# Attention rounds beside Strassen passes: a round's transposes moved from the end of its own unit to the head of the next one, its mix one unit further

## The reference

```python
scores = scale * np.matmul(q_c, k_c.transpose(0, 1, 2, 4, 3))
scores = scores - np.max(scores, axis=-1, keepdims=True)
attn = np.exp(scores)
attn = attn / (np.sum(attn, axis=-1, keepdims=True) + 1e-09)
out = np.matmul(attn, v_c)
...
gate = 1.0 / (1.0 + np.exp(-(x @ w_gate)))      # 512 -> 1536
val = x @ w_val
x = (gate * val) @ w_out                        # 1536 -> 512
...
h = x @ w_in                                    # 512 -> 2048
g = np.where(h >= 1, h, np.where(h <= -1, 0.0, (h + 1) ** 2 / 4))
return g @ w_out                                # 2048 -> 512
```

## Time and profile before

| what | value |
|---|---|
| median of 3 runs | 1626.27 us (1622.51 to 1630.38) |
| the profiled execution, own time | 1621.38 us |
| its span | 1619.5 us |
| granted PE clock, mean | 1.00 |
| PE busy | 1595.8 us (99%) |
| DVE busy | 1138.2 us (70%) |
| ACT busy | 787.5 us (49%) |
| POOL busy | 513.3 us (32%) |

### The profile page before, as it was taken

The page is one execution under the profiler, slowest core; times in us unless marked ns, Lnnn a source line. Parts: engine busy times, 40 slices in busy tenths (PEclk is TensorE's granted clock), DMA queues, the critical chain, the costliest instruction groups (busy, mean ns, idle before and its releaser), DMA issues.

```text
span 1619.5 us, 29171 instructions
## 1 busy us (share of the span) xinstructions
PE 1595.8 (99%) x11174; PEld 1564.2 (97%) x11174; DVE 1138.2 (70%) x1611; ACT 787.5 (49%) x1269; POOL 513.3 (32%) x722
## 2 busy tenths in 40 slices
PE   8999999999999999999999999999999999999999
PEld 7899999999999999999999999999999999999998
DVE  5745667776695777678447579588688688588685
ACT  2222344534353444445334475575575575565663
POOL 7877844565765566566400000000000000000000
PEclk9999999999999999999999999999999999999999
DMA  9889799899999999989977877787778878777775
GB/s 304 290 290 331 265 379 358 311 350 368 328 334 363 344 333 322 353 332 325 349 284 262 284 291 284 248 307 278 261 295 285 275 290 275 282 296 257 258 279 170
DMA packets 135449, 489.50 MB, mean 302 GB/s; under 512 B 14224, under 2 KB 55696, under 8 KB 106256
## 3 DMA queue, kind: packets, MB, share of 16 engines
q1 hardware_dynamic: 106096, 417.24, 73.0%
q0 software_dynamic: 12032, 37.76, 6.0%
q10 hardware_dynamic: 17184, 32.64, 5.7%
HBM read 406.32 MB, written 81.26 MB: 301 GB/s over the span
## 4 chain that ended last, share of the span: by engine, by line
PE 85%; DVE 8%; DMA 3%; issue 2%; ACT 1%; POOL 1%; SPq 0%; DVEq 0%; ACTq 0%
PE banks L890 16%; PE banks L892 15%; PE banks L891 15%; PE banks L912 10%; PE banks L914 10%; PE banks L913 10%; DVE split_lo L1646 3%; PE banks L774 1%; PE banks L776 1%; PE banks L775 1%; PE banks L744 1%; DMA tile_in<-v_dram 1%; PE banks L765 1%; PE banks L753 1%; DMA stage_ab<-w_gate_dram 1%
## 5 line engine op out<-in xcount | busy, mean ns | idle before, releaser
L890 PE MATMUL banks<-combo_hi,ring 128*128 128x384 f32 x1512 | 512.4, 339 | 1.3 <-ACT chain L1174 1.1
L892 PE MATMUL banks<-combo_hi,ring 128*128 128x384 f32 x1512 | 505.5, 334 | 0.0
L891 PE MATMUL banks<-combo_lo,ring 128*128 128x384 f32 x1512 | 505.2, 334 | 0.0
L912 PE MATMUL banks<-split_hi,ring 128*128 128x384 f32 x1092 | 366.8, 336 | 5.9 <-DVE split_lo L1646 5.4
L914 PE MATMUL banks<-split_hi,ring 128*128 128x384 f32 x1092 | 365.1, 334 | 0.0
L913 PE MATMUL banks<-split_lo,ring 128*128 128x384 f32 x1092 | 365.0, 334 | 0.0
L890 PEld LDWEIGHTS banks<-combo_hi,ring 128*128 128x128 f32 x1512 | 283.8, 188 | 4.7 <-ACT chain L1174 1.4
L891 PEld LDWEIGHTS banks<-combo_lo,ring 128*128 128x128 f32 x1512 | 284.0, 188 | 0.0
L892 PEld LDWEIGHTS banks<-combo_hi,ring 128*128 128x128 f32 x1512 | 283.8, 188 | 0.0
L1174 ACT ACTIVATE chain<-banks 128x384 f32<-128x384 f32 x324 | 157.3, 488 | 246.0 <-PE banks L892 244.8
L1646 DVE TENSOR_TENSOR split_lo<-g,split_hi 128x768 fp32r<-128x768 f32 x234 | 237.7, 1020 | 32.3 <-ACT split_hi L1251 30.9
(11 more groups left out here) (131 smaller groups left out, 2130.6 us busy)
## 6 DMA issues: line engine op xcount, KB each, us to landing
ring<-w_out_split SPq DMA_DIRECT2D x119, 1024.0 KB, 5.8
ring<-w_in_split SPq DMA_DIRECT2D x108, 1024.0 KB, 6.3
ring<-w_in_split SPq DMA_DIRECT2D x108, 768.0 KB, 7.9
ring<-w_out_split SPq DMA_DIRECT2D x35, 512.0 KB, 5.7
tile_in<-q_k_dram ACTq DMA_DIRECT2D x43, 384.0 KB, 6.8
w_in_split<-weights SPq DMA_DIRECT2D x36, 256.0 KB, 4.0
x_raw<-x_scratch SPq DMA_DIRECT2D x6, 1536.0 KB, 8.9
out_dram<-y SPq DMA_DIRECT2D x24, 384.0 KB, 6.6
```

The costliest lines, as they stand in the source:

```text
L890: pe.matmul(ps, w_lo, hi, start=first and k == 0, stop=False, skip_group_check=more)
L891: pe.matmul(ps, w_hi, lo, start=False, stop=False, skip_group_check=more)
L892: last = pe.matmul(ps, w_hi, hi, start=False, stop=k == 1, skip_group_check=more)
L912: pe.matmul(ps[:, j, :], w_lo, hi, start=first and k == 0, stop=False, skip_group_check=more)
```

## The change

In a unit u of the passes 0 to 3, PE's list has now at its head: the scores of round u-1, the mix of round u-3 and the transposes of round u-2. Before, it had there the scores of round u-1 and the mix of round u-2, and the transposes of round u-1 between product 3 of the unit before and product 7. On ACT, save_x takes round u-3 in place of u-2 (units 3 to 10), and copy_probs_t round u-2 in place of u-1 (units 2 to 9), both at their old places in the unit. On DVE nothing moves. Two rounds are now under way with probabilities at once, so odd rounds use half of `out_chain2`, which is idle in the units. shift waits for the mix and the save of one round less, and the scores wait for the shift of the round before.

```diff
         def probs_of(a):
-            return early[:, a, 3 * N:4 * N] if a < EARLY else probs[:, :]
+            if a < EARLY:
+                return early[:, a, 3 * N:4 * N]
+            return out_chain2[:, 0, :] if a >= 2 * NR + 8 and a % 2 else probs[:, :]
...
                 elif NR < a < 2 * NR + 8:
                     pe.wait_ge(probs_t_copied, a)
+                elif a > 2 * NR + 8 and a % 8:
+                    pe.wait_ge(shifted, a)
...
                     if attends and u <= 8:
                         scores(round_of(p + 1, u - 1))
+                    if attends and 3 <= u <= 10:
+                        mix(round_of(p + 1, u - 3))
                     if attends and 2 <= u <= 9:
-                        mix(round_of(p + 1, u - 2))
+                        transpose_probs(round_of(p + 1, u - 2))
                     unit(p, u, one)
                     unit(p, u, two)
                     unit(p, u - 1, 4)
                     unit(p, u, three)
                     unit(p, u, four)
                     unit(p, u - 1, 3)
-                    if attends and u <= 8:
-                        transpose_probs(round_of(p + 1, u - 1))
                     unit(p, u, five)
...
-                    if attends and 2 <= u <= 9:
-                        save_x(round_of(p + 1, u - 2))
+                    if attends and 3 <= u <= 10:
+                        save_x(round_of(p + 1, u - 3))
...
-                    if attends and 1 <= u <= 8:
-                        copy_probs_t(round_of(p + 1, u - 1))
+                    if attends and 2 <= u <= 9:
+                        copy_probs_t(round_of(p + 1, u - 2))
...
+                behind = a > 2 * NR + 8 and a % 8 > 0
                 if a > EARLY:
-                    dve.wait_ge(mixed_done, a)
+                    dve.wait_ge(mixed_done, a - behind)
                 if a > 2 * NR:
-                    dve.wait_ge(x_saved, a - 2 * NR)
+                    dve.wait_ge(x_saved, a - behind - 2 * NR)
```

## The result

| | before | changed |
|---|---|---|
| median | 1628.11 us (10 runs) | 1635.97 us (10 runs) |
| range of the runs | 1621.67 to 1631.84 | 1632.19 to 1639.33 |
| profiled execution, own time | 1621.38 | 1637.18 |
| its span | 1619.5 | 1635.4 |
| ratio | | 1.0052, 95% interval 1.0038 to 1.0066 |

The profiled execution of before lies at the fast end of its runs and that of the changed kernel at the slow end of its own, so the 16 us between the two spans are twice the real difference. What follows is told by pieces, not by spans.

A forecast was written before the change was run, and what follows sets the result against it. PE, busy 99% of the span, bounds the kernel. Terms 0 + 1.4 - 0.7 + 6.3 - 0.3 = +6.7 us take the profiled 1621.4 to 1628.1; adding 4.9 to the median gives 1633 us, range 1623 to 1641.

The forecast's parts named there:

- Part 1: PE's 32 groups: transposes joined to scores and mix gain nothing, 0 us, bounds -2.6 to +3.2.
- Part 2: PE, each of four passes: one more entry into the 64x64 form, +1.4 us in all.
- Part 3: PE's transposes: coming later, they no longer wait for normalize, -0.7 us, bounds 0 and -1.2.
- Part 4: Odd units: transposes no longer cover the copy behind tanh12, so mixes at units 4, 6, 8, 10 wait, +6.3 us.
- The waits for v stay: Mixes: v's load keeps its timing and waits stay; overlap with the new copy waits at even units gives -0.3 us.
- v is late: Rival, chance 0.2: v lands 0.3 to 0.4 us later in most of 28 mixes, up to 8 us, 1641 us.
- the signs that I gave it: Marks of late v in the profile: mix waits for v over 5 us, median landing about 7.7 us.
- The first rival: Chance 0.2: transposes' waits go and no copy wait comes at the mixes, -2.4 to +0.2 us, 1625 us.
- the order did what it says: Rival, chance 0.02: PE's list would not show the claimed move at every unit; no size given.

The follow-up runs named there:

- experiment 6: The changed kernel with transposes and their copy back at their old places, only mix and save a unit later, plus a second buffer for v: 1623.15 us, ratio 0.9979.
- experiment 5: The changed kernel with a second buffer for v and the copy of the probabilities ahead of tanh12 on ACT: 1622.48 us, ratio 0.9977.
- experiment 9: v_doubled with the copy of the odd rounds' probabilities made twice on ACT, behind tanh12: 1637.89 us, ratio 1.0066.
- experiment 2: The changed kernel with transposes and their copy back at their old places; only mix and save stay a unit later: 1633.13 us, ratio 1.0040.
- the second profile of before: The kernel before, unchanged, run and profiled once more: 1627.29 us, ratio 0.9999.
- experiment 8: The changed kernel with a second buffer for v of each pass's last round alone, loaded a unit ahead: 1635.27 us, ratio 1.0055.
- v_doubled: The changed kernel with a second buffer for v, used by odd rounds and loaded two units ahead: 1627.85 us, ratio 1.0014.
- cover_back: The changed kernel with the same round's transposes back between product 3 and product 7 in odd units alone: 1634.09 us, ratio 1.0045.

## Why the prediction was right

The forecast was +6.7 us and no change within 0.5%, with a chance of 0.34 for more; it is +8.5 by the first measurement and +7.3 by the second, on the edge between the two. By its steps:

- **Part 1, joining (0).** Slightly better: 0.06 us gained for a group, some -2 us over the 32, within the bounds. The transposes carry hardly any entry or exit of their own.
- **Part 2, one more pair of changes of form (+1.4).** The groups cost what the rows said, scores alone and mix alone 0.71 each. The rule of the Trainium skill (TensorEngine Tiling (Array Packing), Key Properties: a change of mode drains TensorE) fits, as the transposes joined to a mix saved only 0.06 of the 0.35 that a pair costs. That the 1.4 stands in the time was not shown: experiment 6 could not tell it from the late copies that go.
- **Part 3, the transposes' waits (-0.7).** Gone, as said.
- **Part 4, the lost cover (+6.3).** Right in place and size: 0.30 where 0.29 was said and 0.70 where 0.70, a price of 6.0 us by experiment 5, and a slope near one by experiment 9, each with 3 to 4 us left open by the intervals. One detail was wrong: at unit 6 I put the wait on top of the lateness of before in every pass. In the first profile the mix is 0.30 late there in the passes 0 and 2, like the others, and 0.83 in pass 1; what tile_sums adds comes and goes.
- **"The waits for v stay", with -0.3 for overlap.** This is the term that failed. With v's waits taken out of both kernels, 0.34% or 5.5 us of the change are left (1.0014 against 0.9980, with 3.4 open to either side). The other parts as now measured give 6.0 + 1.4 - 0.7 - 2 - 1 for the late copies of before, about 4, within the error. The remaining 2 to 3 us of the 8 are put down to waits for v that the change adds. The times alone do not show that, since it is no more than the error; the starts of the mixes (later by v by 7 us in the two profiles of the changed kernel, by 2.2 and 5.3 in those of before) and experiment 2 against 6 do. The rival "v is late" had the right resource, as an addition, but not its price of 8 us. By the signs that I gave it, it came too: waits for v over 5 us (6.0 and 6.7) and a median landing near 7.7 (7.6 and 7.7). The signs do not tell the cases apart, as the second profile of before has 4.4 and 7.6.

That the sum came within 2 us is in part luck: v was put some 3 us too low, and joining (-2 against 0) and the copies that were late before (-1, which stood in no term) made up for it.

The first rival (waits go and none comes) fell, and the order did what it says.

**What stays open.** Why the later mix meets v worse, though v is issued at the same point of a unit, is needed by the next mix as before, and lands in the same median time. Profiles point to the last round of a pass, whose v is issued and needed a unit later than before; experiment 8, which took that wait away, did not get faster. And the share of v in the changed kernel cannot be added to that of the copy: taking the copy away is worth 1.5 us with one buffer for v and 6.0 with two; taking v away is worth 6 us with the copy held up and over 10 without it (1.0043 to 0.9977).

Three versions beat both kernels, the one before by 0.2%, and cannot be told from each other: the kernel before with a second buffer for v (0.9980), the mix one unit later with it (0.9979), and the changed kernel with it and the copy ahead of tanh12 (0.9977).

## What to carry to other kernels

Before work is moved out of a stretch of the bounding engine, look at what other engines do in that stretch: if their chain is as long as the engine's own way, the moved work was its cover, and its length comes back as a wait; here 0.33 us moved made 0.30 us of wait, to be seen beforehand from a margin of 0.04. When an instruction waits for two things that are both nearly late, repair of one can show next to nothing (1.5 us here, and 6.0 with the other gone), so take one away for good before pricing the other. Moving the consumer of a copy later helps only if the copy does not move with it: in mix_late_v_doubled, where the copy kept its unit, no mix waited for it, and in v_doubled, where it moved along and stood behind tanh12 again, sixteen did.

## What the runs showed of the hardware

A long stall of PE can cost more than itself. Behind the wait of 4.2 us for the ring in the changed kernel, nine steps between matmuls were 0.32 us, not 0.173. PE's timeline there, from the wait to the step at which the pace is back:

```profile
212.64 0.67 PE L895 MATMUL banks<-combo_hi,ring 128*128 128x384 f32 x1 [4.20 <-DMA ring<-w_in_split]
213.11 0.52 PE L896 MATMUL banks<-combo_lo,ring 128*128 128x384 f32 x1
213.43 0.52 PE L897 MATMUL banks<-combo_hi,ring 128*128 128x384 f32 x1
213.75 0.52 PE L895 MATMUL banks<-combo_hi,ring 128*128 128x384 f32 x1
...
215.99 0.40 PE L896 MATMUL banks<-combo_lo,ring 128*128 128x384 f32 x1
216.23 0.34 PE L897 MATMUL banks<-combo_hi,ring 128*128 128x384 f32 x1
216.41 0.33 PE L895 MATMUL banks<-combo_hi,ring 128*128 128x384 f32 x1
```

and the stretches before, at and after it (columns as in the earlier trace rows):

```profile
207.00:212.00 5.00, 1.44 (x30) 0.89 (x28) 2.81 (x5) 0.94 (x2) 3.10 (x4) 1.00 1.03 419
212.00:216.40 4.40, 3.76 (x12) 3.76 (x13) 0.00 (x0) 0.91 (x2) 1.08 (x2) 0.61 1.03 424
216.40:221.00 4.60, 4.60 (x28) 4.60 (x28) 2.64 (x7) 0.87 (x2) 2.83 (x5) 1.00 0.74 295
```

The granted clock fell to 0.61 of full speed in the mean of the second stretch, where the steps are those of the lower of the two levels, 1.2 GHz, and it was back at 2.4 GHz in the third. The twelve steps from 212.64 to 216.41 took 3.77 us where 2.08 is usual, 1.7 us on top of the wait. The wait of 5.2 us in v_last_early has the same nine steps of 0.32 behind it. The waits of 0.3 to 0.7 us for the copy left the steps at 0.173. Around 2 us the runs show both: in the changed kernel a wait of 2.0 us for v, at 531.5, had no slow step behind it, and in cover_back one of 2.1 us for split_lo, at 460.1, had nine of 0.32 (granted clock 0.51 from 460.0 to 463.5).
